# Layer one's attention steps in another order, and the product of k and v per head

## What is computed

```python
def _attn_ref(q, k, v):                      # each (4, 8, 576, 64)
    q_s = np.exp(q - np.max(q, axis=-1, keepdims=True))
    q_s = q_s / (np.sum(q_s, axis=-1, keepdims=True) + 1e-09)
    k_s = np.exp(k - np.max(k, axis=2, keepdims=True))
    k_s = k_s / (np.sum(k_s, axis=2, keepdims=True) + 1e-09)
    kv = np.einsum('bhsd,bhse->bhde', k_s, v)
    return np.einsum('bhsd,bhde->bhse', q_s, kv)

# x = attention, as (2304, 512)
# layer one:  h = x @ w_in;  g = s * relu(h)**2 + b;           x = g @ w_out
# layer two:  h = x @ w_in2; g = h * tanh(log1p(exp(h)));      out = g @ w_out2
```

## Time and profile before

| | before |
|---|---|
| runs | 889.14, 889.38, 892.09 us (median 889.38) |
| the profiled execution | 890.38 us, its span 888.6 us |
| PE busy | 865.1 us, 97% of the span |
| DVE busy | 613.5 us, 69% |
| ACT busy | 378.7 us, 43% |
| POOL busy | 26.6 us, 3% |
| layer one with attention (T = 0 to 2) | from about 40 to 339 us |

### The profile page before, as it was taken

The page is one execution under the profiler, slowest core; times in us unless marked ns, Lnnn a source line. Parts: engine busy times, 40 slices in busy tenths (PEclk is TensorE's granted clock), DMA queues, the critical chain, the costliest instruction groups (busy, mean ns, idle before and its releaser), DMA issues.

```text
span 888.6 us, 11126 instructions
## 1 busy us (share of the span) xinstructions
PE 865.1 (97%) x4132; PEld 717.5 (81%) x4132; DVE 613.5 (69%) x1037; ACT 378.7 (43%) x621; POOL 26.6 (3%) x30
## 2 busy tenths in 40 slices
PE   9789999999999999999999899998999999999998
PEld 4578888888888888888997678897888788878886
DVE  8787776665475554222466889688797779778975
ACT  4445433332333323222356555455454445445443
POOL 2300000000000000000000000000000000000000
PEclk9799999999999999999999999999999999999999
DMA  9921111111111100000153000100000000000001
GB/s 227 339 53 40 25 29 28 41 41 41 41 40 40 40 0 1 1 1 0 49 190 143 1 0 1 48 1 1 25 1 0 12 36 0 0 28 19 0 0 48
DMA packets 60645, 36.15 MB, mean 41 GB/s; under 512 B 48320, under 2 KB 50368, under 8 KB 60608
## 3 DMA queue, kind: packets, MB, share of 16 engines
q1 hardware_dynamic: 60608, 35.66, 14.2%
HBM read 30.93 MB, written 4.72 MB: 40 GB/s over the span
## 4 chain that ended last, share of the span: by engine, by line
PE 80%; DVE 11%; ACT 6%; issue 2%; POOL 1%; DMA 0%; DVEq 0%; ACTq 0%
PE H L796 38%; PE Y L810 21%; PE Y L824 17%; PE H L763 2%; PE H L784 2%; ACT t L458 1%; DVE g L702 1%; DVE t L674 1%; ACT t L460 1%; DVE wout_lo L598 1%; DVE t L679 1%; ACT wout_hi L360 1%; DVE t L684 1%; PE H L775 1%; DVE win_lo L598 1%
## 5 line engine op out<-in xcount | busy, mean ns | idle before, releaser
L796 PE MATMUL H<-xs_hi,win_hi 128*128 128x512 f32 (+1 forms) x640 | 240.8, 376 | 7.7 <-DVE g_raw L697 3.3
L796 PE MATMUL H<-xs_hi,win_lo 128*128 128x512 f32 (+1 forms) x640 | 236.8, 370 | 0.0
L796 PE MATMUL H<-xs_lo,win_hi 128*128 128x512 f32 (+1 forms) x640 | 236.7, 370 | 0.0
L824 PE MATMUL Y<-wout_hi,g 128*128 128x512 f32 x576 | 190.1, 393 | 5.4 <-DVE g L702 5.4
L810 PE MATMUL Y<-g,wout_hi 128*128 128x512 f32 (+1 forms) x640 | 183.3, 371 | 0.7 <-DVE g L582 0.7
L796 PEld LDWEIGHTS H<-xs_hi,win_hi 128*128 128x128 f32 x640 | 121.4, 190 | 30.0 <-DVE g_raw L697 4.0
L796 PEld LDWEIGHTS H<-xs_hi,win_lo 128*128 128x128 f32 x640 | 121.3, 190 | 20.8
L796 PEld LDWEIGHTS H<-xs_lo,win_hi 128*128 128x128 f32 x640 | 121.4, 190 | 20.4
L824 PEld LDWEIGHTS Y<-wout_hi,g 128*128 128x128 f32 x576 | 108.7, 189 | 30.9 <-DVE g L702 8.7
L810 PEld LDWEIGHTS Y<-g,wout_hi 128*128 128x128 f32 x640 | 115.2, 189 | 20.1 <-DVE g L582 0.9
L577 DVE SCALAR_TENSOR_TENSOR g_raw<-g_raw,s_col 128x512 f32<-128x512 f32 (+1 forms) x80 | 55.5, 694 | 96.4 <-ACT g_raw L381 96.1
(11 more groups left out here) (73 smaller groups left out, 823.2 us busy)
## 6 DMA issues: line engine op xcount, KB each, us to landing
win_raw<-in_moe_w_in_dram SPq DMA_DIRECT2D x8, 1024.0 KB, 7.0
wout_raw<-in_moe_w_out_dram SPq DMA_DIRECT2D x8, 1024.0 KB, 7.3
g_flat<-in_v_dram SPq DMA_DIRECT2D x32, 144.0 KB, 3.3
out_dram<-xy SPq DMA_DIRECT2D x18, 256.0 KB, 2.1
qbuf<-in_q_dram SPq DMA_DIRECT2D x24, 144.0 KB, 2.8
kbuf<-in_k_dram SPq DMA_DIRECT2D x24, 144.0 KB, 2.9
raw<-in_k_dram SPq DMA_DIRECT2D x4, 288.0 KB, 3.9
raw<-in_q_dram SPq DMA_DIRECT2D x4, 288.0 KB, 6.1
```

The lines of the kernel that those rows point to most:

```text
L796: last = nc.tensor.matmul(Hb[f % banks][:, 0:w], a[:, i, cols], m[:, i, 0:w], start=(i == 0 and n == 0), stop=(i == KC - 1 and n == XPASS ...
L824: last = nc.tensor.matmul(Y[i][:, :], g[:, f % LAG_B, a, rows], m[:, f, :], start=(f == 0 and n == 0), stop=(f == FC - 1 and n == XPASS - 1))
```

## The change

The change has four parts. First, kv_product makes one result per head: 12 matmuls of 64 stationary and 65 moving columns in the place of 6 of 128 and 130. Head 0 goes to PSUM partitions 0 to 63 and head 1 to 64 to 127, both in columns 0 to 64, and kv_norm reads the sums with one instruction in the place of two. Second, on DVE the steps q_max, q_shift and k_max of a unit stand behind square and g_lo of step i = 0, not ahead of them, and the rest follows: k_shift stands between square and g_lo of i = 1, and q_sum to q_scale behind g_lo of i = 1, where they stood behind g_lo of i = 0. Third, on ACT q_exp stands in step i = 1, between relu and g_hi, where it stood behind g_hi of i = 0. Fourth, the ACT split of the second quarter of w_in is moved from ahead of tile 0 to behind g_hi(0) of it.

```diff
-        FIRST_HI = {2: ('out', 1), 4: ('in', 2), ...
+        FIRST_HI = {0: ('in', 1), 2: ('out', 1), 4: ('in', 2), ...
...
             wout_hi_part(0, 0)
-            win_hi_part(0, 1)
             act.wait_ge(sb_in, 32)
...
                     relu(T, f, w)
+                    if attention and i == 1:
+                        q_exp(n)
                     if attention and i == 2:
                         take_qT(n)
                     g_hi(T, f, w)
-                    if attention and i == 0:
-                        q_exp(n)
                     if attention and i == 1:
                         k_exp(n)
...
-                for h in range(PAIR):
-                    rows = slice(h * D, (h + 1) * D)
-                    last = nc.vector.tensor_scalar_add(ksum[rows, n.p, :], bank[rows, (h + 1) * VW - 1:(h + 1) * VW], EPS)
+                last = nc.vector.tensor_scalar_add(ksum[:, n.p, :], bank[:, VW - 1:VW], EPS)
...
-                    last = nc.vector.tensor_scalar(kv[rows, n.p, h * D:(h + 1) * D], bank[rows, h * VW:h * VW + D],
+                    last = nc.vector.tensor_scalar(kv[rows, n.p, h * D:(h + 1) * D], bank[rows, 0:D],
...
+                    if attention and i == 1 and p:
+                        take_x(Unit(T + 1, p - 1))
+                    if attention and i == 3:
+                        kv_norm(n)
+                    square(T, f, w)
+                    if attention and i == 1:
+                        k_shift(n)
+                    g_lo(T, f, w)
+                    if attention and i == 1:
+                        q_sum(n)
+                        q_eps(n)
+                        q_inv(n)
+                        q_scale(n)
                     if attention and i == 0:
                         q_max(n)
                         q_shift(n)
                         k_max(n)
-                    if attention and i == 1:
-                        if p:
-                            take_x(Unit(T + 1, p - 1))
-                        k_shift(n)
-                    if attention and i == 3:
-                        kv_norm(n)
-                    square(T, f, w)
-                    g_lo(T, f, w)
...
-                    if attention and i == 0:
-                        q_sum(n)
-                        q_eps(n)
-                        q_inv(n)
-                        q_scale(n)
...
                 for j in range(J):
-                    last = nc.tensor.matmul(n.bank[0][:, 0:PAIR * VW], n.kj[:, j, :], n.v[:, :, j, :],
-                                            start=(j == 0), stop=(j == J - 1))
+                    for h in range(PAIR):
+                        rows = slice(h * D, (h + 1) * D)
+                        last = nc.tensor.matmul(n.bank[0][rows, 0:VW], n.kj[:, j, rows], n.v[:, h, j, :],
+                                                start=(j == 0), stop=(j == J - 1))
```

More of the change, by code:

```diff
@@ L164, in linear_attention_moe_kernel @@
         SPLIT_ORDER = [(w, layer, i) for layer in range(2) for i in range(NG) for w in ('in', 'out')]
-        FIRST_HI = {2: ('out', 1), 4: ('in', 2), 6: ('out', 2), 8: ('in', 3), 10: ('out', 3)}
+        FIRST_HI = {0: ('in', 1), 2: ('out', 1), 4: ('in', 2), 6: ('out', 2), 8: ('in', 3), 10: ('out', 3)}
         FIRST_LO = {1: ('in', 1), 3: ('out', 1), 5: ('in', 2), 7: ('out', 2), 9: ('in', 3), 11: ('out', 3)}
```

## The result

The changed kernel takes 903.05 us (median of 4 runs, 901.35 to 903.68), beside 890.74 us for the kernel before (median of 4 runs, 889.14 to 893.13). The ratio is 1.0133, with a 95% interval of 1.0102 to 1.0164: it is slower by about 12 us. The profiled execution has a span of 901.2 us, 12.6 more than before.

The account below looks back on a forecast made before the run. PE, busy for 97% of the span, was taken as the bound. 7.3 + 0.65 + 4.5 + 1.8 - 3.0 = +11.2 on 890.4 gives 901.6, median 900.6 us; 8-in-10 range 894.0 to 907.0.

Parts of the forecast that it names:

- The start of tile 1: PE waits 3.56 us at q_transpose for DVE's q_scale; with 0.1 for weights, twice (tiles 1 and 2), 7.3 us lost.
- The walk: DVE's steps in the new order, timed one after another from profiled durations, to find when q_scale ends against PE's arrival.
- The start of tile 0: PE's 2.9 us relu wait shrinks to 0.9, a 4.3 us wait for q_scale comes; transposes 0.65 us late.
- The clock: TensorE at half clock behind each of the three new waits in layer one: 1.5 us each, 4.5 in all (3 to 5.1).
- Units 1 to 3: Middle units of each tile: q_scale's slack all gone, 0.2 us lost in each of 9 units, 1.8 us (0 to 3.2).
- The product: kv_product per head with half the possible overlap: 1.1 us against 1.35, 0.25 saved in each of 12, 3.0 us in all.
- The rival without overlap: In kv_product the heads' halves don't overlap, or small matmuls are issue-bound: saves nothing or costs up to 4.9, 903.6 to 908.5; 32%.
- The rival of a whole overlap: In kv_product the heads' halves overlap wholly, saving 8.1 us, waits as walked: 895.5; 20%, of it half below 893.8.
- the most likely band: Layer one's waits as walked, with a product in between (1.0 to 1.25 us): 898.5 to 903, chance 42%.

Follow-up runs that it names:

- The unit 0 experiment: Changed kernel with DVE's and ACT's old order put back in unit 0 of tiles 1 and 2 alone: 890.68 us, ratio 0.9989 to the kernel before.

## Why the prediction was right

Forecast were 900.6 us and a range of 894.0 to 907.0; the median is 903.05.

- **The start of tile 1.** The walk gave a wait of 3.56 us, and the row has 3.43 idle. From the last matmul of the four ups to the transposes of tile 2 (261.28 to 265.10) are 3.82 us, 3.59 more than the 0.23 that such a step takes. This was the largest term and came within 0.1 us in each tile. The unit 0 experiment shows that it decides the result.
- **The start of tile 0.** Relu's wait was to shrink to 0.9 us and is 0.7; q's was to be 4.3 and is 4.0; the transposes were to start 0.65 us later than before and start 0.85 later. Of that 0.2 are from the stage ahead, where DVE was ready at 46.38 and not at 46.16.
- **The clock: right in kind, too small in size.** The term "I charge 1.5 each, 4.5 us in all" was read from two places of the trace before, where the loss was 1.5 and 1.7. It measured 2.5, 1.6 and 2.7, that is 6.8 us, above the 5.1 given as its upper end. Two waits of the same length, 3.43 us, were followed by 1.6 and 2.7, and in the experiment with the heads one after the other the third wait, also of 3.43, was followed by none. Over the 16 waits for the scaling of q in the traces of the changed kernel and of five experiments (all of 3.4 to 5.1 us), the way from the transposes to the product took 5.9 to 6.1 us ten times, 5.0 five times and 3.40, the time at full clock, once. So the wait's length alone doesn't set the loss; both samples of before were of the shorter kind. The work put into the waits shows that the term is the clock's. What decides between no slow stretch, a short one and a long one stays open.
- **Units 1 to 3.** Forecast were 0.2 us each for all the slack used up. In unit 3 of tile 2, from the last matmul ahead of the transposes to the first behind them are 0.85 us (338.51 to 339.36), where they were 0.67 (325.23 to 325.90): 0.18 us. In unit 1 of the three tiles it is 0.17 to 0.19.
- **The product.** 1.1 us was taken, with a saving of 0.25 each and 3.0 in all; the saving is 0.31 each and 3.7 in all, so by the forecast's own count the product is at 1.04 (1.35 - 0.31). From its start to the next matmul it went from 1.26 to 0.85, and half of 1.26 would be 0.63: about two thirds of the possible overlap came, and the step from the last matmul ahead of a product to the product is 0.09 us longer. The rival without overlap is out by that row. The rival of a whole overlap is out too, since it would have saved 8.1 us. The 1.1 itself was the middle between two bounds and no mechanism, so it is luck that it came so near. Of the two rules of the Trainium skill on tiling ("TensorEngine Tiling (Array Packing)", Key Properties), the one on parallel tiles agrees with the rows; whether the 0.09 us is the drain of a change of mode, no run here shows. By the 62 ns a matmul of the Trainium skill, "TensorE: Matmul & The Clock Gate", Part 1, a product would take 1.49 us, an estimate for hardware decoding switched off; the 24 records took 0.85, so that limit isn't in force here.

Sum again, with what was measured, up to the last product: 0.85 + 7.2 (two waits of 3.6) + 6.8 + 1.6 (nine of 0.18) - 3.7 = 12.8, beside the 13.2 of the table. Layer two then gives 0.6 back. It is one slow stretch: behind a wait of 1.9 us the kernel before ran at half clock for a while, and the changed kernel behind the same wait did not (4.88 us from 617.64 to 622.52, beside 4.29 from 630.84 to 635.13).

So the mechanism was right where the forecast put most of it, in the waits at unit 0, and the total is near since the terms that were too small (the clock by 2.3 us, the start of tile 0 by 0.2) are partly made up by the product's 0.7 and layer two's 0.6. The time alone would have misled: 903.05 lies between the most likely band (898.5 to 903) and the one for no overlap (903 to 908.5), whose mechanism the rows exclude. What took it there is the clock.

## What to carry to other kernels

A step that waits for nothing is worth most where its engine is about to be idle: q_max filled DVE's time ahead of the first strip, and put behind that strip it was late by the whole idle time and all that queued with it. So cost a moved step at the place where its consumer has the least slack (here the first unit of a tile, where PE has no down between its ups), not in the steady state, where the same move cost 0.2 us a unit. And a wait of 3 to 5 us on TensorE costs another 1.5 to 2.8 us through the clock behind it in nearly all of these traces, which the waits of about 1 us in layer one did not. Last, when an engine is late, read in the program every semaphore that it waits for: behind the wait that was taken away the next one stood ready, the copy of the transposed q.

## What the runs showed of the hardware

- Matmuls on different halves of the array's columns overlap with their neighbours in the queue, and the order decides: the same 24 records took 0.85 us with the heads by turns and 1.37 with one head after the other. With one head after the other and both results on one half they took 1.54. Whether the halves decide, or the place in PSUM that the neighbours add to, is not shown.
- After waits of the same length, 3.43 us, TensorE's granted clock stayed at 1.2 GHz for different times, with 1.6 and 2.7 us lost, and once did not fall at all. Behind a wait of 1.9 us it fell in one trace and not in another.
- Matmuls whose result nobody reads, put into the waits, kept the granted clock at 2.4 GHz and made the kernel 6.3 us faster.
